# A linear-attention, channel-mix and MLP chain on one core: the program written out without engine loops, with three pieces of its schedule moved

## The reference

```python
for t in range(S):                                   # attention with a decaying state
    state = alpha[:, :, t, :, None] * state + np.einsum('bhd,bhe->bhde', k[:, :, t], v[:, :, t])
    y[:, :, t] = np.einsum('bhd,bhde->bhe', q[:, :, t], state)
x = y.transpose(0, 2, 1, 3).reshape(B, S, H * D)
xk = mu_k * x + (1.0 - mu_k) * x_prev                # x_prev: x one token earlier
xr = mu_r * x + (1.0 - mu_r) * x_prev
k = np.maximum(xk @ w_k, 0.0)                        # 384 -> 1024
x = sigmoid(xr @ w_r) * ((k * k) @ w_v)              # 1024 -> 384
u = x + (x.transpose(0, 2, 1) @ U @ V).transpose(0, 2, 1)    # rank 32 over the tokens
out = u + np.maximum(u @ w_ch1, 0.0) @ w_ch2         # 384 -> 1536 -> 384
```

## Time and profile before

| | |
|---|---|
| median of 3 runs | 855.51 us (853.7 to 856.09) |
| the profiled execution | 855.14 us, its span 853.4 us |
| PE busy | 788.8 us (92%), 10680 matmuls |
| DVE, ACT, POOL busy | 423.9, 272.7, 71.6 us |
| mean granted TensorE clock | 0.962 |
| instruction queue of PE (q8) | 88 packets, 1.44 MB |

### The profile page before, as it was taken

One profiled execution on the slowest core, in us unless ns is written; L12 is line 12 of the kernel. 1 busy time (PEld: TensorE's weight loads), 2 busy tenths in 40 slices (PEclk: granted clock), 3 DMA queues, 4 the chain that ended last, 5 costly groups with the idle time before them and its releaser, 6 DMA issues.

```text
span 853.4 us, 24863 instructions
## 1 busy us (share of the span) xinstructions
PE 788.8 (92%) x10680; PEld 732.5 (86%) x10680; DVE 423.9 (50%) x752; ACT 272.7 (32%) x555; POOL 71.6 (8%) x141
## 2 busy tenths in 40 slices
PE   5768888989999998998999998998999999999998
PEld 5767777969999897978999898896999989979998
DVE  4658658652377315753176524665147622433122
ACT  1542543242423323233242414223333333421121
POOL 3421101100011000100001100110001100000000
PEclk9978996999999998999999999899999999998999
DMA  7660040001200041000300013000220000000000
GB/s 218 202 234 3 18 118 2 2 15 55 66 30 4 15 111 37 3 2 23 110 30 2 16 55 94 2 3 15 68 81 2 2 21 2 28 2 1 1 28 28
DMA packets 15603, 37.33 MB, mean 44 GB/s; under 512 B 2544, under 2 KB 6512, under 8 KB 15504
## 3 DMA queue, kind: packets, MB, share of 16 engines
q1 hardware_dynamic: 15408, 35.72, 14.2%
q10 hardware_dynamic: 96, 0.07, 0.0%
HBM read 29.89 MB, written 4.72 MB: 41 GB/s over the span
## 4 chain that ended last, share of the span: by engine, by line
PE 80%; DVE 10%; issue 5%; ACT 2%; DMA 2%; SPq 0%; DVEq 0%; ACTq 0%
PE acc L617 11%; PE acc L619 11%; PE acc L618 11%; PE hps L617 10%; PE hps L618 9%; PE hps L619 9%; PE aps L442 7%; PE aps L506 3%; PE aps L549 2%; DVE QK L1069 2%; PE hps L705 2%; DVE Pm L1042 1%; PE aps L533 1%; PE acc L442 1%; DVE hid_h L1169 1%
## 5 line engine op out<-in xcount | busy, mean ns | idle before, releaser
L1214 DVE SCALAR_TENSOR_TENSOR hid_l<-hps,hid_h 128x384 fp32r<-128x384 f32 x96 | 53.5, 557 | 216.1 <-ACT hid_h L942 216.1
L942 ACT ACTIVATE hid_h<-hps 128x384 fp32r<-128x384 f32 x96 | 47.2, 492 | 208.0 <-PE hps L619 208.0
L1069 DVE TENSOR_TENSOR QK<-QK,T 112x768 f32<-112x768 f32 x96 | 91.4, 964 | 35.2 <-PE aps L442 31.9
L617 PE MATMUL hps<-in_h,w_h 128*128 128x384 f32 x288 | 100.5, 349 | 1.0 <-DVE in_l L1190 0.9
L1325 POOL TENSOR_TENSOR T<-T 112x384 f32<-112x384 f32 (+5 forms) x96 | 51.8, 543 | 560.2 <-DVE QK L1052 310.0
L442 PEld LDWEIGHTS aps<-QK 48*64 48x64 f32 x4704 | 77.0, 138 | 24.5 <-issue 24.3
L619 PE MATMUL hps<-in_h,w_l 128*128 128x384 f32 x288 | 97.0, 337 | 0.0
L618 PE MATMUL hps<-in_l,w_h 128*128 128x384 f32 x288 | 97.0, 337 | 0.0
L619 PE MATMUL acc<-w_h,hid_l 128*128 128x384 f32 x288 | 96.4, 335 | 0.0
L617 PE MATMUL acc<-w_h,hid_h 128*128 128x384 f32 x288 | 96.3, 334 | 0.0
L618 PE MATMUL acc<-w_l,hid_h 128*128 128x384 f32 x288 | 96.2, 334 | 0.0
(11 more groups left out here) (149 smaller groups left out, 1340.7 us busy)
## 6 DMA issues: line engine op xcount, KB each, us to landing
QK<-in_k SPq DMA_DIRECT2D x16, 336.0 KB, 4.2
QK<-in_q SPq DMA_DIRECT2D x16, 336.0 KB, 4.5
T<-in_alpha SPq DMA_DIRECT2D x16, 336.0 KB, 5.0
raw<-in_w_ch SPq DMA_DIRECT2D x6, 768.0 KB, 6.6
out<-x SPq DMA_DIRECT2D x24, 192.0 KB, 1.9
vt<-in_v SPq DMA_DIRECT2D x8, 288.0 KB, 4.4
QK<-in_v SPq DMA_DIRECT2D x7, 288.0 KB, 2.8
raw_k<-in_w_k SPq DMA_DIRECT2D x3, 512.0 KB, 4.9
```

Source lines behind the costliest of these rows:

```text
L617: pe.matmul(o, a[0], b[0], start=first, stop=False)
L942: nc.scalar.activation(hid[0][:, f % 2, :], hps[f % 2][:, 0:HT], ACT.Relu).then_inc(s_rel2, 1)
L1069: nc.vector.tensor_tensor(qk, qk, t, ALU.mult).then_inc(s_qk[g], 1)
L1214: nc.vector.scalar_tensor_tensor(out=hid[1][:, f % 2, :], in0=hps[f % 2][:, 0:HT], scalar=0.0, in1=hid[0][:, f % 2, :].bitcast(F32), op0=A ...
```

## The change

1. All `Fori` loops (PE, ACT, DVE, POOL, SP) are replaced by Python loops: the program is written out, every wait is against a constant, and the `nop` with `s_go` at the attention tiles is gone. The wider waits of the loop on DVE go too.
2. `BESIDE1` is shifted: the diagonal runs at place 1 in place of 0, and the level l = 5, until then at place 8, at place 9 (levels 0 to 4 each move to the next place in use).
3. In DVE's `token_mix` the level l = 6 scaling of Q and K runs after the first three u additions.
4. In DVE's first `channel_mix` the gate of half 0 runs inside the mix that followed ahead of it (after its second tile).
5. SP issues `move_split(0, 0)` and the load of v ahead of the loads of `w1` and `w2`; `w1` waits for all six split DMAs.
6. The low parts of the second piece of `wk` and `wv` move from DVE to POOL; `LOWS` is cut accordingly.

```diff
             sp.wait_ge(s_a2[0], 16)
+            sp.wait_ge(s_a2[1], 16)
+            move_split(0, 0)
+            sp.wait_ge(s_y[0], 2)
+            load_v(0, 1, 0)
+            sp.wait_ge(s_split, 32 * KT)
             load_part(w1w, w_ch1, 0, 1, s_w1[0])
-            sp.wait_ge(s_a2[1], 16)
             load_part(w1w, w_ch1, 1, 1, s_w1[1])
             sp.wait_ge(s_w1[0], 16)
             load_part(w1w, w_ch1, 2, 1, s_w1[2])
-            move_split(0, 0)
-            sp.wait_ge(s_y[0], 2)
-            load_v(0, 1, 0)
...
-                    if g == 0 and not (isinstance(n, int) and n < 2):
+                    if g == 0 and n >= 2:
                         pe.wait_ge(s_x[1], 2 * n)
-                    pe.nop().then_inc(s_go, 1)
...
-            with pe.Fori(0, NB - 1) as b:
+            for b in range(NB - 1):
...
                         dve.wait_ge(s_lv[g], LV * n + l + 1)
-                        if g == 0 and not fixed:
-                            dve.wait_ge(s_lv[1], LV * n + l + 1)
...
                 step(plan[1 + F1])
-                before_last()
+                finish()
+
+            def gate(b, half):
...
-                step(plan[1])
                 for c in range(NC):
                     if c == HC:
-                        step(plan[2])
+                        step(plan[1] + plan[2])
                         low_u(b, 0)
...
-                for i in range(1, NK):
+                for i in range(2, NK):
                     for n in (NR + i, NR + NK + i):
                         low(n)
                         yield
...
-            channel_mix(0, 0, step, FIRST, lambda: mix(0, 1, 0))
+            channel_mix(0, 0, step, FIRST, lambda: mix(0, 1, 0, lambda: gate(0, 0)))
...
+                def finish():
+                    low_u(b, 1)
+                    gate(b + 1, 0)
...
-            for n in (*range(NR + 1), NR + NK):
-                low(n, n)
+            for n in (*range(NR + 1), NR + NK, NR + 1, NR + NK + 1):
+                low(n)
...
-BESIDE1 = [1, 1, 1, 0, 1, 1, 0, 1, 1, 0]
+BESIDE1 = [0, 1, 1, 0, 1, 1, 0, 1, 1, 1]
...
-LOWS = [0, 1, 1, 1, 1, 1, 1, 0, 1, 1, 1, 1, 2]
+LOWS = [0, 1, 1, 1, 1, 0, 0, 0, 1, 1, 1, 1, 2]
```

More of the change, by code:

```diff
@@ L154, in unit @@
         def unit(n):
-            return units[n] if isinstance(n, int) and n < 2 else units[2]
+            return units[min(n, 2)]
         def opens(n):
-            return isinstance(n, int) and n == 0
+            return n == 0
         acc = [pb(f"acc{i}") for i in range(3)]
@@ L225, in ge @@
         def ge(eng, s, n):
-            if isinstance(n, int) and n <= 0:
-                return
-            eng.wait_ge(s, n)
+            if n > 0:
+                eng.wait_ge(s, n)
         def pieces():
@@ L254, in wk_low @@
         def wk_low(eng, i):
-            if i == 0:
-                eng.wait_ge(s_plo, NR + 1)
+            if i < 2:
+                eng.wait_ge(s_plo, NR + 2 * i + 1)
             else:
-                eng.wait_ge(s_vlo, 2 * i - 1)
+                eng.wait_ge(s_vlo, 2 * i - 3)
         def wv_low(eng, i):
-            if i == 0:
-                eng.wait_ge(s_plo, NR + 2)
+            if i < 2:
+                eng.wait_ge(s_plo, NR + 2 * i + 2)
             else:
-                eng.wait_ge(s_vlo, 2 * i)
+                eng.wait_ge(s_vlo, 2 * i - 2)
         def mask_at(lev):
@@ L274, in own_banks @@
         def own_banks(b, half):
-            return half == 0 or isinstance(b, int)
+            return half == 0 or b == NB - 1
         def u_bank(b, half, j):
@@ L300, in loaded @@
         def loaded(eng, n, s, g):
-            if isinstance(n, int) and n == 1:
+            if n == 1:
                 eng.wait_ge({s_ldq[g]: s_q2, s_ldk[g]: s_k2, s_lda[g]: s_a2}[s[g]][g], 16)
@@ L411, in _ @@
             load_rest(1, 0)
-            with sp.Fori(0, NB - 2) as b:
+            for b in range(NB - 2):
                 load_v(b + 1, 0, 1)
@@ L657, in channel_mix @@
                 src_r, src_k = inp[half], inp[1 - half]
-                first = isinstance(b, int) and s == 0
+                first = opens(s)
                 step(plan[0])
@@ L744, in mlp @@
                     if f == 0 and half == 0:
-                        pe.wait_ge(s_vlo, 2 * NK - 2 + 2 * N1)
+                        pe.wait_ge(s_vlo, 2 * NK - 4 + 2 * N1)
                     if f >= 2:
@@ L996, in _ @@
             last_weights()
-            with act.Fori(0, NB - 1) as b:
+            for b in range(NB - 1):
                 steps = attention(b + 1, 0)
@@ L1044, in levels @@
             def levels(n):
-                fixed = isinstance(n, int)
                 u = unit(n)
@@ L1070, in levels @@
                         if l < ML:
-                            if g == 0 and fixed:
+                            if g == 0:
                                 dve.wait_ge(s_lv[1], LV * n + l + 1)
@@ L1159, in mix, with channel_mix @@
                 low(KT - 1)
-            def channel_mix(b, half, step, plan, before_last=lambda: None):
+            def channel_mix(b, half, step, plan, finish):
                 s = 2 * b + half
@@ L1174, in channel_mix @@
                 step(plan[1 + F1])
-                before_last()
+                finish()
+            def gate(b, half):
+                s = 2 * b + half
                 dve.wait_ge(s_sig, HC * (s + 1))
@@ L1253, in _ @@
             dve.wait_ge(s_const, 6 + ML)
-            steps = together(attention(0, 1), lows(), LOWS, 2 * NK - 2 + N1)
+            steps = together(attention(0, 1), lows(), LOWS, 2 * NK - 4 + N1)
             step = stepper(steps)
@@ L1257, in _ @@
             mix(0, 0, 0)
-            channel_mix(0, 0, step, FIRST, lambda: mix(0, 1, 0))
+            channel_mix(0, 0, step, FIRST, lambda: mix(0, 1, 0, lambda: gate(0, 0)))
             run(steps)
             last_lows()
-            with dve.Fori(0, NB - 1) as b:
+            for b in range(NB - 1):
                 steps = attention(b + 1, 0)
                 step = stepper(steps)
-                channel_mix(b, 1, step, BESIDE1)
+                channel_mix(b, 1, step, BESIDE1, lambda: gate(b, 1))
                 token_mix(b, step, BESIDE_T)
@@ L1269, in _ @@
                 step = stepper(steps)
-                channel_mix(b + 1, 0, step, BESIDE1, lambda: low_u(b, 1))
+                def finish():
+                    low_u(b, 1)
+                    gate(b + 1, 0)
+                channel_mix(b + 1, 0, step, BESIDE1, finish)
                 mlp(b, 1, step, BESIDE3, lambda: mix(b + 1, 1, 0))
@@ L1273, in _ @@
             b = NB - 1
-            channel_mix(b, 1, alone, BESIDE1)
+            channel_mix(b, 1, alone, BESIDE1, lambda: gate(b, 1))
             token_mix(b, alone, BESIDE_T)
@@ L1326, in attention, with low @@
                     yield
-            def low(n, hi):
+            def low(n):
                 src, w_hi, w_lo = PIECES[n]
-                pool.wait_ge(s_whi, hi + 1)
+                pool.wait_ge(s_whi, n + 1)
                 nc.gpsimd.tensor_tensor(w_lo, src, w_hi.bitcast(F32), ALU.subtract).then_inc(s_plo, 1)
             run(attention(0))
-            for n in (*range(NR + 1), NR + NK):
-                low(n, n)
-            pool.wait_ge(s_plo, NR + 2)
+            for n in (*range(NR + 1), NR + NK, NR + 1, NR + NK + 1):
+                low(n)
+            pool.wait_ge(s_plo, NR + 4)
             pool.wait_ge(s_vst, 2)
@@ L1342, in _ @@
             run(attention(1))
-            with pool.Fori(1, NB) as b:
+            for b in range(1, NB):
                 run(attention(2 * b))
```

1 line of the change is left out of this document (removed).

## The result

The changed kernel took 825.48 us, the median of four executions (819.44 to 827.21); the kernel before, timed beside it, took 854.61 (852.13 to 856.09). The ratio is 0.9649, 95% interval 0.9594 to 0.9705.

What follows compares the result with a forecast made beforehand. PE, busy 92% of the span, was taken as the bound, with time to gain from its idle gaps, its clock and its waits for other engines. Terms summed to 20.1 us off 855.14, giving 835.0 us, range 826 to 844.

Steps and rivals of the forecast that it cites:

- prologue (2.7 + 0.7 + 1.5): Before the loop: split ahead of w1 saves 2.7 us, low parts to POOL 0.7, gate inside the mix 1.5.
- half 0, three times (3 x 0.47 - 2.0): Half 0 channel mixes: 0.47 us saved each at the add of f = 1, 2.0 lost in all at their ends.
- half 1, twice (11.4 + 2 x 0.47): Half 1 channel mixes: 11.4 us saved at two loop ends, plus 0.47 each at the add of f = 1.
- Loop ends: Where PE jumps back and waits for code: no loops and a later diagonal save 5.7 us each, bounds 2.9 and 7.2.
- f = 1: PE's wait ahead of that add: l = 0 replacing l = 1 at place 2 saves 0.47 us in five halves, 2.3 together.
- End of half 0: l = 5 at place 9 queues ACT's copies ahead of u's high parts: 0.65 us lost each, 2.0 over three.
- Token mix, the step that failed: Scaling behind the u additions cuts PE's wait from 2.40 to 1.23 us: 3.5 saved over three; clock gain taken as 0.
- Rival A: Shorter gaps keep the clock high in three token mixes (5 us) and behind the first half (3): 827 us; chance 17%.
- Start: Split issued ahead of w1: ACT's first mix starts near 50.6 us, saving 2.7 us, bounds 1.5 and 3.4.
- The low parts and the gate: Prologue: two low parts moved to POOL save 0.7 us (0 to 1.8), gate inside the mix 1.5 (0 to 4).
- B: DVE, late for the l = 0 and l = 2 tiles, costs 1.2 us in each of six halves: 842 us; chance 18%.
- D: Straight code not fetched in time, 1.53 us per miss where small tiles follow closely; 25 misses give 873 us; chance 3%.

Runs made afterwards that it cites:

- experiment 1: The kernel before with its five engine loops written out, nops and wide waits kept: 836.14 us, ratio 0.9796.
- experiment 3: The change with the old BESIDE1 (diagonal at place 0, l = 5 at place 8), run twice: 821.51 and 821.92 us, ratios 0.9648 and 0.9645.
- experiment 2: The kernel before written out, with the nops at the attention tiles removed and the wide waits narrowed: 835.49 us, ratio 0.9791.
- experiment 5: The change with the split again behind w1's pieces: 827.85 us; the kernel before, written out, with the split ahead of them: 836.88 us.
- experiment 6: The change with the two low parts back on VectorE and the first gate behind the whole mix again: 823.11 us, ratio 0.9662.
- experiment 8: The change with unused products while TensorE awaits first loads: 824.50 us; also one ahead of each of 14 level steps of the first unit: 830.64 us.
- experiment 7: The change with four unused products in each token-mix gap (first kernel): 825.25 us; also ahead of the two first r products (second): 827.67 us.

## Why the prediction was right, and where it was wrong

The direction and the main cause held: PE stood at the loop's end because of the loop, most likely for code behind the jump, and the clock fell behind that. The sizes were short. With the means of the three profiles of before and the two of the change:

| part | priced | measured |
|---|---|---|
| prologue (2.7 + 0.7 + 1.5) | 4.9 | 175.0 - 168.6 = 6.4 |
| three token mixes | 3.5 | 46.6 - 40.1 = 6.5 |
| half 0, three times (3 x 0.47 - 2.0) | -0.6 | 263.3 - 263.3 = 0.0 |
| half 1, twice (11.4 + 2 x 0.47) | 12.3 | 195.2 - 181.9 = 13.3 |
| last stretch | 0 | 167.9 - 167.5 = 0.4 |
| sum | 20.1 | 26.6 |

- **Loop ends.** 5.7 each was forecast for the shift of the first hidden product, and the saving up to that stage was 5.7 and 5.8 in the pair first compared (r at 1.04 us behind the last addition, as said). That the figure fits is partly luck, since it held two parts of opposite sign: writing out is worth 6.6 (experiment 1), the new places take 0.6 back (experiment 3).
- **f = 1.** The gap went, worth 0.6 where 0.47 was priced, but mostly for another reason than the one given: 0.33 of it was gone with VectorE's wide wait alone (experiment 2). The prediction didn't list that wait among what the change removes.
- **End of half 0.** A loss, as priced at 0.65 each, but more: 1.0 from the last addition to the mlp. It was made up by f = 1 (0.6) and smaller pieces, and that half 0 came out even, near the -0.6 priced, is luck.
- **Token mix, the step that failed.** "In the last token mix a 1.23 us gap did not prevent a fall, so I take 0": the order itself saved 1.15, as priced, and the clock added 1.45 wherever it stayed high, which was in 17 of 24. One row of one token mix was taken for a rule, and that mix is not like the others: in the last one PE stands twice for 1.23 us, ahead of the products with V and ahead of the transposes, in the loop only 0.37 and 1.23. This term, put at 0, is 3.0 us of the 6.5 missing. Rival A had it at 5 and named the right place; it should have carried part of the sum. The Trainium skill (TensorE: Matmul & The Clock Gate, Part 4: PE-mode transpose) says that transposes don't count as activity for the clock; the prediction concluded that with nine of them behind the gap the 0 was certain. The trace doesn't agree with that conclusion: in the second token mix of the change they run at 1.00, and the level holds.
- **Start.** ScalarE's first mix came at 48.05, not 50.6, but in that pair of profiles 4.3 us of the difference is the first unit, which ended that much earlier with the same work in it, and only 1.0 the wait behind it. Over all profiles the order is worth 3.8, against 2.7 and an upper bound of 3.4, and in the timed medians 0 to 2.4 (experiment 5). The low parts and the gate brought nothing (experiment 6).
- **The base.** The sum was made against a profiled execution of 855.14 us. The three of this kernel average 853.3, and 32 timed ones in the later comparisons lie around medians of 852.3 to 852.8. Some 2 to 3 us of the 9.5 are this, and the 26.6 of the table is to be set beside 27 (852.5 less 825.5), not beside 29.1. No term for the spread between executions stood in the range.
- **Rivals.** B would have shown as new waits of PE for VectorE in six halves; the only one is at the end of half 0. D: the written-out program fetches 84 packets of code, the kernel before 88, where the prediction reckoned over a hundred from one stretch; no stall stands in the loop, and those of the prologue (experiment 1) stood there before. By the Trainium skill (Runtime: NRT & Kernel Launch, Instruction fetch mechanics) fetches of straight code hide behind a floor of time per instruction; the trace agrees that they are hidden in the loop, not in the prologue, and shows no such floor: 75 pairs of instructions in 1.32 us.

**What stays open:** why the clock falls at different moments in the prologue of one program (the kernel before had 3.4 us at the low level behind 130 us in one profile and 10.2 in two), and whether the stands for code in the prologue have a part in it; why the last token mix kept its level in both profiles of experiment 3, the change with the old places, but in none of the thirteen others without fillers in the token mix, six of which have the old places too; and the size of the split's part.

## What to carry to other kernels

Price the clock as a term with a chance, not as 0 or 1: here the level fell in 21 of 21 token mixes with a gap of 2.40 us, in 7 of 24 with 1.23, and in none of nine where products without a use filled the gap to 0.34. They must be no longer than the gap. Before pricing a change from one profile, look how far two executions of the same program lie apart in each stretch; here a pass of the written-out loop repeats to 0.1 us, falls of the clock apart, and the first 180 us differ by up to 7.7. And price each edit alone even when rows give their sum: the written-out loop hid that the new places cost 1.3 us per pass.

## What the runs showed of the hardware that was not expected

- The first unit of this kernel runs at the low level, though the page prints 1.00 for it: there is no record of the clock before its first rise (38.9 us in the change, 45.4 in the kernel before). Where fillers forced an earlier record (experiment 8), the same stretch reads 0.51, and its tiles are no slower than in the change. The pace says the same: 48 small products in 1.50 us at the start of the change's timeline, 96 in 1.60 in the loop.

```profile
5.80 1.50 PE L441 MATMUL acc<-QK 48*64 48x32 f32 x48 [5.80 <-DMA QK<-in_q]
552.13 1.60 PE L441 MATMUL aps<-QK 48*64 48x32 f32 x96
```

(the second row is from the first kernel of experiment 7; the length of so short a group includes the modelled end of its last product, so the pace is read from starts: 26 to 28 ns from one to the next against 14.5)

- A token mix with gaps of 0.37 and 1.23 us takes 12.9 us in one pass and 14.3 to 14.4 in another, with not one instruction changed. Only the fall of the clock differs.
- Straight code is not always there in time: with the loop gone, PE still stands 1.2 to 1.9 us for "issue" in the prologue, a code packet just ahead of the stand, where the DMA engines moved 298 GB/s (40 to 50 us of experiment 1); the loop has no such stand.
- Three SyncE transfers of the split, 1.9 us on a quiet queue, held ScalarE 9.4 us when three pieces of w1 were issued ahead of them (experiment 5), and 4.6 us in the kernel before, which has the same order.
